# A three-part transformer layer on one core: a reordered head with wider and constant TensorE products, the token softmax moved into the last group, and half of one expert's second matrix loaded into another buffer

## What is computed

```
for t in range(S):                                   # 8 heads of 48, 4 batches
    cur = einsum('bhd,bhe->bhde', u * k[t], v[t])
    y[t] = einsum('bhd,bhde->bhe', r[t], state + cur)
    state = w[t][..., None] * state + einsum('bhd,bhe->bhde', k[t], v[t])
x = y as (3072, 384)
h = x @ w_in; x = (h * clip(h + 3, 0, 6) / 6) @ w_out   # 384 -> 2048 -> 384
logits = x @ phi                                     # 32 slots, 4 for each of 8 experts
d = softmax of logits over the tokens; slot_input = d.T @ x
slot_out[e] = relu(slot_input[e] @ w1[e]) @ w2[e]    # 384 -> 1024 -> 384
c = softmax of logits over the slots; out = c @ slot_out
```

## Time and profile before

| | |
|---|---|
| median of 3 runs | 452.84 us (452.33 to 454.29) |
| profiled execution, its time / its span | 455.68 us / 454.0 us |
| TensorE busy | 427.3 us (94%), mean granted clock 0.946 |
| VectorE busy | 340.9 us (75%) |
| GpSimd busy | 180.1 us (40%) |
| ScalarE busy | 148.4 us (33%) |
| moved by DMA | 69.35 MB |

### The profile page before, as it was taken

How to read it: one execution, slowest core, us unless ns; L and a number is a source line. 1 busy time by engine, 2 the same in 40 slices (tenths; PEclk the granted TensorE clock), 3 DMA queues, 4 the chain that set the end, 5 groups by cost and what they waited for, 6 DMA issues and landing times.

```text
span 454.0 us, 9636 instructions
## 1 busy us (share of the span) xinstructions
PE 427.3 (94%) x3891; PEld 238.2 (52%) x3891; DVE 340.9 (75%) x539; ACT 148.4 (33%) x250; POOL 180.1 (40%) x174
## 2 busy tenths in 40 slices
PE   7999997888999999999999999998999999999982
PEld 3898654444555555556555555464554534433420
DVE  7555589989998989888898998889776676472233
ACT  1221323542433334414344144342432323212122
POOL 5614255575544565446556435654370000000000
PEclk9555699999999999999999999999999999999987
DMA  8996130341933222340343213330005963469919
GB/s 215 300 381 223 61 115 1 115 113 64 337 107 114 77 70 83 115 116 11 104 116 113 86 31 114 114 114 18 37 2 206 423 222 124 181 250 423 395 62 359
DMA packets 15245, 69.35 MB, mean 153 GB/s; under 512 B 2016, under 2 KB 2656, under 8 KB 13152
## 3 DMA queue, kind: packets, MB, share of 16 engines
q1 hardware_dynamic: 15200, 68.73, 43.7%
HBM read 64.00 MB, written 4.72 MB: 151 GB/s over the span
## 4 chain that ended last, share of the span: by engine, by line
issue 39%; PE 33%; POOL 19%; DVE 4%; DMA 1%; ACT 1%; POOLq 0%; SPq 0%; DVEq 0%
POOL att L1256 5%; PE hid L514 4%; PE hid L516 4%; PE hid L515 4%; POOL att L1228 4%; POOL att L1226 3%; POOL att L1241 3%; POOL att L1274 3%; PE hid L711 2%; PE l_ps L570 2%; PE l_ps L544 2%; PE y_ps L471 2%; PE sc_ps L421 1%; PE hid L686 1%; PE sc_ps L686 1%
## 5 line engine op out<-in xcount | busy, mean ns | idle before, releaser
L1123 ACT ACTIVATE relu<-hid,three 128x512 f32<-128x512 f32 x96 | 65.9, 687 | 149.6 <-PE hid L516 149.0
L514 PE MATMUL hid<-x_split,w_split 128*128 128x512 f16 x288 | 109.9, 381 | 3.5 <-DVE gated L860 3.5
L515 PE MATMUL hid<-x_split,w_split 128*128 128x512 f16 x288 | 109.6, 380 | 0.0
L516 PE MATMUL hid<-x_split,w_split 128*128 128x512 f16 x288 | 109.4, 380 | 0.0
L860 DVE SCALAR_TENSOR_TENSOR gated<-relu,hid 128x512 f32<-128x512 f32 x96 | 65.2, 680 | 29.6 <-ACT relu L1123 29.0
L870 DVE STREAM_TRANSPOSE ring<-gated 128x512 f32<-128x512 f32 x96 | 68.3, 711 | 3.3
L1247 POOL TENSOR_TENSOR att<-att 128x1024 f16<-128x1024 f32 x20 | 39.9, 1996 | 64.6 <-ACT att L1082 64.6
L1265 POOL TENSOR_TENSOR att<-att 112x512 f32<-112x512 f32 x19 | 24.3, 1280 | 68.7 <-DVE att L785 68.7
L514 PEld LDWEIGHTS hid<-x_split,w_split 128*128 128x128 f16 x288 | 28.3, 98 | 40.8 <-issue 9.6
L516 PEld LDWEIGHTS hid<-x_split,w_split 128*128 128x128 f16 x288 | 28.2, 98 | 34.4 <-issue 0.5
L515 PEld LDWEIGHTS hid<-x_split,w_split 128*128 128x128 f16 x288 | 28.2, 98 | 25.2 <-issue 0.6
(11 more groups left out here) (202 smaller groups left out, 768.7 us busy)
## 6 DMA issues: line engine op xcount, KB each, us to landing
att<-nat_dram SPq DMA_DIRECT2D x20, 576.0 KB, 4.2
att<-rkT_dram SPq DMA_DIRECT2D x22, 448.0 KB, 5.6
att<-w_dram SPq DMA_DIRECT2D x5, 1536.0 KB, 14.1
att<-wT_dram SPq DMA_DIRECT2D x22, 226.2 KB, 4.7
out_dram<-w_split SPq DMA_DIRECT2D x12, 384.0 KB, 3.9
stage<-w_in_dram SPq DMA_DIRECT2D x2, 1536.0 KB, 13.7
ring<-w_outT_dram SPq DMA_DIRECT2D x1, 3072.0 KB, 17.2
stage<-w_dram SPq DMA_DIRECT2D x2, 1536.0 KB, 9.2
```

Source lines behind the costliest of these rows:

```text
L514: pe.matmul(hid[s % 2][:], high, x_high, start=(q == 0), stop=False)
L515: pe.matmul(hid[s % 2][:], high, x_low, start=False, stop=False)
L516: last = pe.matmul(hid[s % 2][:], low, x_high, start=False, stop=(q == KT - 1))
L1123: nc.scalar.activation(relu_tile(s), hid[s % 2][:], ACT.Relu, bias=three[:], scale=GATE / H_SCALE)\
```

## The change

1. **Head.** The 16 opening constant products become 10, 4 and 3, the last two lots behind `suffix_done` and `prefix_done`. `diagonal` writes each of its products 48 times side by side (96 columns in place of 2), `attend_first` takes two heads' columns per product (96 in place of 48; the second half is overwritten by the next product). `stay_warm` stands three times in each unit (2, 1 and 1 products). `turn_x` goes ahead of `increment`, `diagonal` behind `attend_first`. `make_fold` goes from VectorE to ScalarE, `scan_suffix(5)` and `low_w(0)` go ahead of step 0.
2. **Group 0.** Pieces 2 to 7 of `low_w` go from VectorE to GpSimd, behind a new ScalarE operation `scale_w` that scales the stage in place.
3. **Softmax c.** Units 0 to 19 (640 of 768 columns) are done inside group 5: maximum and sums on VectorE, subtraction, multiplication and low part on GpSimd, exponential and high parts on ScalarE; `turn_c(1)` and `turn_c(0)` run at steps 96 and 97 in place of six of nine `stay_warm` products. Units 20 to 23 and `turn_c(2)` stay in the tail.
4. **Tail.** Both `pick_slots` stand behind the whole `apply_w2`; the first half of w2[4] is loaded into `x_late` right behind w1[6]; `weigh` computes the weights ahead of alpha.

```diff
+            elif e == 4 and a < EK // 2:
+                home, first = x_late, a * DM
...
-        def split_at(s):
-            return s // 2 + 1 if s % 2 == 0 and s // 2 + 1 < W_PIECES else None
+        def scaled_behind(s):
+            return {0: 3, 4: 4, 5: 5, 8: 6, 9: 7}.get(s)
+
+        def split_behind(s):
+            return {1: 2, 2: 3, 5: 4, 6: 5, 9: 6, 10: 7}.get(s)
...
+            sp.dma_start(x_late, w2[4][:, 0:UNIT // 2]).then_inc(w2_late_in[0], 16)
             sp.wait_ge(l_ready, STEPS)
...
-                for e in (4, 6, 7):
+                for e in (6, 7) if half == 0 else (4, 6, 7):
...
-                    last = pe.matmul(hid[1][:, 2 * p:2 * p + 2], rk_prod[n % 2][0:PD, p * P:(p + 1) * P],
-                                     u_rows[0:PD, 2 * p:2 * p + 2], start=True, stop=True, skip_group_check=True)
+                    last = pe.matmul(hid[1][:, p * 2 * D:(p + 1) * 2 * D].rearrange("p (o j) -> p o j", j=2),
+                                     rk_prod[n % 2][0:PD, p * P:(p + 1) * P],
+                                     u_rows[0:PD, 2 * p:2 * p + 2].rearrange("p (o j) -> p o j", o=1)
+                                     .broadcast_to([PD, D, 2]), start=True, stop=True, skip_group_check=True)
...
-                        cols = slice((2 * p + j) * D, (2 * p + j + 1) * D)
+                        h = 2 * p + j
+                        cols = slice(h * D, min(h + 2, H) * D)
...
-            for _ in range(16):
-                pe.matmul(hid[0][:, :], warm[:, 0:P], warm[:, P:P + GT], start=True, stop=True, skip_group_check=True)
+            keep_awake(10)
+            pe.wait_ge(suffix_done, 1)
+            keep_awake(4)
+            pe.wait_ge(prefix_done, 1)
+            keep_awake(3)
             score(0, None)
+            turn_keys(0)
...
+            stay_warm(2, hid[0])
             diagonal(0)
             for n in range(B):
                 if n:
                     score(n, None)
-                turn_keys(n)
+                    turn_keys(n)
+                stay_warm(2, hid[0])
+                attend_first(n)
                 if n + 1 < B:
                     diagonal(n + 1)
-                else:
-                    stay_warm(2, hid[0])
-                attend_first(n)
+                stay_warm(1, hid[0])
+                turn_x(n)
                 increment(n, None)
-                turn_x(n)
                 stay_warm(1, hid[0])
...
-                    stay_warm(6, y_ps)
+                    pe.wait_ge(c_lo_done, 1)
+                    pe.wait_ge(c_hi_done, 2)
+                    turn_c(1)
+                    pe.wait_ge(gated_done, STEPS - 1)
+                    stay_warm(3, hid[0])
                 if s == STEPS + 1:
-                    stay_warm(3, y_ps)
+                    turn_c(0)
...
-            pe.wait_ge(c_lo_done, 1)
-            turn_c(0)
             apply_w2(0, 1)
-            turn_c(1)
+            pe.wait_ge(c_lo_done, 2)
+            pe.wait_ge(c_hi_done, 4)
             turn_c(2)
...
             apply_w2(1, 0)
-            pick_slots(0)
             pe.wait_ge(w2_late_in[1], 48)
             apply_w2(1, 1)
-            pick_slots(EG - 1)
+            for g in range(EG):
+                pick_slots(g)
...
+                if n == 2:
+                    low_w(0)
             low_x(B - 1)
-            low_w(0)
+            scan_suffix(B + 1)
+            restart_prefix(B + 1)
             mask_first(B)
...
+                if s == STEPS - 12:
+                    cols, tiles = c_parts[0]
+                    dve.wait_ge(logits_done, C - 1)
+                    nc.vector.tensor_reduce(cmax[:, tiles], by_slot(soft[:, cols]), AX_X, ALU.max).then_inc(c_max_done, 1)
+                if s == STEPS - 8:
+                    c_inverse(0)
+                if s == STEPS:
+                    copy_cT(1)
+                    copy_cT(0)
...
+            def scale_w(c):
+                act.wait_ge(w_hi_done, c + 1)
+                nc.scalar.activation(stage[:, c * WP:(c + 1) * WP], stage[:, c * WP:(c + 1) * WP], ACT.Copy,
+                                     scale=W_IN_SCALE).then_inc(w_scaled, 1)
...
+                if s == STEPS - 10:
+                    c_exp(0)
+                if s == STEPS - 5:
+                    c_high(0)
...
+            def low_w(c):
+                pool.wait_ge(w_scaled, c - 1)
+                per = FT // W_PIECES
+                nc.gpsimd.tensor_tensor(w16[:, c * per:(c + 1) * per, 1].rearrange("p i q m -> p i (q m)"),
+                                        stage[:, c * WP:(c + 1) * WP].rearrange("p (i n) -> p i n", i=per),
+                                        w16[:, c * per:(c + 1) * per, 0].rearrange("p i q m -> p i (q m)"),
+                                        ALU.subtract).then_inc(w_lo_rest_done, 1)
```

More of the change, by code:

```diff
@@ L289, in build_program @@
         c_lo_done = sem("c_lo_done")
-        c_turned = sem("c_turned")
+        c_turned = [sem(f"c_turned{n}") for n in range(3)]
+        c_max_done = sem("c_max_done")
+        c_inv_done = sem("c_inv_done")
         cT_done = sem("cT_done")
@@ L533, in stay_warm, with keep_awake @@
                               skip_group_check=True)
+            def keep_awake(n):
+                for _ in range(n):
+                    pe.matmul(hid[0][:, :], warm[:, 0:P], warm[:, P:P + GT], start=True, stop=True,
+                              skip_group_check=True)
             def add_logits(g, m):
@@ L558, in natural_logits, with turn_c @@
                 last.then_inc(nat_logits_ready, 1)
+            def turn_c(n):
+                for i in range(8 * n, 8 * n + 8):
+                    last = pe.transpose(c_bank[n][0:3 * SLOTS, :].bitcast(F16)[:, i % 8 * P:(i % 8 + 1) * P],
+                                        c_split[:, i].rearrange("p a s -> p (a s)"), ident16_sb[:])
+                last.then_inc(c_turned[n], 1)
             def gather_slots(g, n):
@@ L609, in _ @@
                     weigh_phi(0)
+                if s == 1:
                     increment(B, s)
@@ L700, in turn_eh @@
                         last.then_inc(eh_turned, 1)
-            def turn_c(n):
-                for i in range(8 * n, 8 * n + 8):
-                    last = pe.transpose(bank[1 + n][0:3 * SLOTS, :].bitcast(F16)[:, i % 8 * P:(i % 8 + 1) * P],
-                                        c_split[:, i].rearrange("p a s -> p (a s)"), ident16_sb[:])
-                last.then_inc(c_turned, 1)
             def apply_w2(g, half):
@@ L902, in sum_weight @@
                     nc.vector.tensor_reduce(run_sum, weight, AX_X, ALU.add).then_inc(run_sum_done, 1)
-            def make_fold():
-                for q in range(4):
-                    block = ident[SLOTS * q:SLOTS * (q + 1), SLOTS * q:SLOTS * (q + 1)]
-                    last = nc.vector.tensor_copy(
-                        fold[SLOTS * q:SLOTS * (q + 1), :].rearrange("p (c s) -> p c s", c=4),
-                        block.rearrange("p (o s) -> p o s", o=1).broadcast_to([SLOTS, 4, SLOTS]))
-                last.then_inc(fold_made, 1)
             def add_slots(g):
@@ L955, in _ @@
                 g, i = divmod(s, FT)
+                if s <= 1:
+                    gate(s)
+                    turn_gated(s)
                 if phase == 0:
@@ L980, in _ @@
                 if s == 0:
-                    gate(0)
-                    turn_gated(0)
                     low_w(1)
-                    scan_suffix(B + 1)
-                    restart_prefix(B + 1)
+                    sum_diag(B)
                 if phase == 3:
@@ L1053, in _ @@
                     .then_inc(ehT_done[0], 1)
[L1054 to L1058 removed]
+            copy_cT(2)
             low = slice(2 * SLOTS, 3 * SLOTS)
@@ L1106, in high_x, with make_fold @@
                     .then_inc(x_hi_done, 1)
+            def make_fold():
+                for q in range(4):
+                    block = ident[SLOTS * q:SLOTS * (q + 1), SLOTS * q:SLOTS * (q + 1)]
+                    last = nc.scalar.activation(
+                        fold[SLOTS * q:SLOTS * (q + 1), :].rearrange("p (c s) -> p c s", c=4),
+                        block.rearrange("p (o s) -> p o s", o=1).broadcast_to([SLOTS, 4, SLOTS]), ACT.Copy)
+                last.then_inc(fold_made, 1)
             def high_w(c):
@@ L1174, in _ @@
                         copy_keys(n)
-                c = split_at(s)
-                if c is not None and c >= 2:
-                    high_w(c)
                 if s < STEPS:
@@ L1181, in _ @@
                     copy_keys(B)
+                c = scaled_behind(s)
+                if c is not None:
+                    high_w(c)
+                    scale_w(c)
                 if g >= 1 and i == 2:
@@ L1290, in _ @@
             nc.gpsimd.memset(three[:], 3.0 * GATE).then_inc(pool_consts, 1)
-            decay_keys(0)
-            multiply_rows(0)
             for b in range(B):
@@ L1296, in _ @@
             last.then_inc(state_zeroed, 1)
-            multiply_rows(1)
+            decay_keys(0)
```

(8 more changed lines are left out.)

159 lines of the change are left out of this document (98 added, 61 removed).

## The result

The changed kernel takes 432.12 us (431.88 to 432.25, four runs), the kernel before 452.72 (452.33 to 454.29) beside it: a ratio of 0.9538, 95% interval 0.9515 to 0.9561. The forecast was 429.0 in a range of 422 to 443. The profiled execution takes 432.12 (span 430.4), where the sum gave 431.5.

The account below looks back on a forecast made before the run. The prediction took TensorE, at half clock, to bound the head and VectorE's share of the split group 0. Terms 12.8 + 1.3 + 8.0 + 2.1 = 24.2 us, off the median 452.84, gave 429, range 422 to 443.

Parts of the forecast that it names:

- The time goes into loading weights, not into columns: Head, TensorE: 2 and 48 columns cost the same 0.22 us per instruction, so wider products were costed at nothing.
- rivals 1 and 2: Head's clock: first, up only in part, 438 us, chance 0.14; second, at half throughout, 448 us, chance 0.09.
- (c): Head: at full clock the chain over VectorE and GpSimd, not TensorE, sets the pace, 6.9 us a unit.
- (d): Head from its data-fixed start: `finish_y(0)` at 15.1, step 0 at 38.5 instead of 51.34; 12.8 us gained.
- (e): Step 0's first products: about six run at half clock before the clock rises; at full clock 1.3 us more gained.
- Group 0: Split pieces moved from VectorE to GpSimd: three units at 13.2 instead of 15.87 us, 8.0 us gained (5 to 9).
- A piece of over 2 us: Group 0, sign of being wrong: a GpSimd piece of the split taking over 2 us; 1.5 was expected.
- the second delays `decay_keys`, whose result is read a unit later: Group 0, GpSimd: of two pieces per unit, 3.0 us together, the second only holds up `decay_keys`, needed a unit later.
- Rival 3: Group 0: GpSimd becomes the bound, by pieces of 2.1 us or more or mutual blocking with scans; 437 us, chance 0.04.
- Groups 1 to 5: Softmax work placed beside group 5 costs nothing: taken as 0, bounds 0 and 1 us lost.
- tail: After step 95: 1.1 us from `turn_c`, 0.8 from `pick_slots`, 0.2 from weights ahead of alpha; 2.1 us gained.
- the fourth rival: After step 95: clock falls since turning products do not hold it, some 5 us lost; 434 us, chance 0.05.

Follow-up runs that it names:

- narrow: The change with the diagonal's products back at 2 columns and the first attention's at 48, added constant products kept: 442.9, 434.44, 447.41 and 444.05 us.
- order only: The change with narrow products and the head's constant products as before, leaving only the new order of the head: 445.36 us, ratio 0.9798 to the kernel before.
- fewer: The change with the head's constant products as in the kernel before, wide products and order kept: 432.03 us, ratio 0.9513 to the kernel before.
- Experiment 11: Also called `low_v_first`: the change with `low_v` ahead of `low_x` and `sum_diag` in group 0; median 431.11 us, ratio 0.9502 to the kernel before.
- experiment 8: The change without the three constant products at step 96 and the nine ahead of the gather: 433.03 us, ratio 0.9513 to the kernel before.
- Experiment 7: The change with the first half of w2[4] loaded late again, into the stage: 433.54 us, ratio 0.9529 to the kernel before.
- experiment 1: The kernel before, unchanged, profiled a second time: 455.79 us profiled, span 454.1.
- experiment 6: The change with each unit's second `low_w` piece one place later on GpSimd, behind `decay_keys`: 436.98 us, ratio 0.96 to the kernel before.

## Why the prediction held, and where it was off

**The bound and the clock.** "The time goes into loading weights, not into columns" held: in the first unit, at full clock, the attention took 1.88 us in the change and 1.88 in narrow, the diagonal 1.13 and 1.05. The clock stayed up in the head of all nine traces with wide products, and fell in both with narrow ones (445 us for order only), near what rivals 1 and 2 say. The constant products that were added gave nothing measurable beside the wide ones, and cost nothing either, since TensorE is not the bound there: the 0.29 by which `fewer` reaches step 0 sooner stand already in its first scan (3.71 and 3.99), which waits for a transfer. The forecast gave them no price of their own, so no term failed with it.

**(c), the chain over VectorE and GpSimd.** That TensorE does not set the pace is shown by `fewer`; that this chain does, by its rows, which add up to the period. The forecast 6.9 was 6.6. Its hand-overs were right (0.11 of the 6.9, 0.09 measured); too high was the end of the chain, where it put `scan_prefix` and `diag_values` one behind the other, 1.22 + 0.83 = 2.05 after `multiply_rows`. The scan starts before `multiply_rows` ends (25.69 and 26.03), and `diag_values` is over 1.72 after it. The forecast named the scan as the operation that waits for GpSimd; it does, by 0.2 (1.44), and then `diag_values` waits for the scan (1.76 instead of 0.83).

(d) had the path of the start wrong. It let `decay_keys(0)` release the next scan at 8.34; in the change the chain runs over the first scans and `decay_receptance(0)` to `multiply_rows(0)` at 8.31. `finish_y(0)` came at 14.64 instead of 15.1; over the eleven traces with the new order it stands at 14.14 to 14.65. The head gave 1.0 us above its 12.8: 0.5 from this start, 0.6 from the two periods, and 0.1 less behind the last `finish_y`. The forecast named a DMA as the last wait in the head as a sign of being wrong. At its very start two transfers are that (1.49 and 1.70 us), as in the kernel before; behind them none is, though the DMA share stood at 9 tenths in the second and third slices.

**(e).** 0.9 instead of 1.3. Step 0's first six products took 2.35 us before (51.34 to 53.69) and 1.30 after (37.51 to 38.81), 1.05 less, since five and not six ran at half clock. The other 0.2 wasn't looked for.

**Group 0: the term that was mis-sized**, 6.4 for 8.0. GpSimd's piece took 1.63 to 1.65 us, the estimate was 1.5. A piece of over 2 us was to be a sign of being wrong; the first took 2.58 (50.26 to 52.84, a scan of VectorE beside it until 51.39), ahead of these three units. The step that failed is not that price, but "the second delays `decay_keys`, whose result is read a unit later": it looked at what waits behind the piece on GpSimd, and not at what runs beside it on VectorE. `low_v` was in its way, and TensorE waits for `low_v`. Experiment 11 gives 0.97 us of the 1.6 back. The rest, 0.2 a unit, is not this wait: 40.27 / 3 = 13.4 with TensorE never waiting. The 13.20 was one interval, and it stood across the end of group 0 (after the change that interval is 13.57, and the next four are 17.80, 13.12, 13.08 and 14.13), so it was a weak measure of a unit that TensorE bounds; why a unit of group 0 takes 0.2 more than it stays open. Rival 3, in its second form ("the scans and the pieces block each other"), was true in small.

**Groups 1 to 5, tail.** 0.35 for 0, and 2.2 for 2.1. The softmax beside group 5 cost nothing: from the last `low_scores` to step 95's end it is 54.56 us in both traces (335.95 to 390.51, 314.52 to 369.08). In the tail 0.2 of the gain is there when `apply_w1` begins (19.82 and 19.63 us behind step 95's end), as forecast for the weights, and 2.0 come behind it, for the forecast's 1.1 and 0.8. Of the fourth rival only the fall of the clock was seen, without constant products (experiment 8); the rule on turning products which the forecast quotes is neither borne out nor refuted. Experiment 7 shows that without the early half load 1.4 of the tail's 2.2 would be lost.

**From the sum to the median.** The sum for the profiled execution was off by 0.6 of span (24.2 for 23.6). The forecast of 429 was 3 us low since the same sum was taken off the median, 452.84. That step failed: the profiled execution of before lies high in a wide spread (452.2 to 456.3), the change's runs lie within 0.6 us. The spread may come from the stretch at half clock: narrow, where the clock falls too, spreads over 13 us (mean clock 0.946 to 0.983, the highest in its shortest run), the change and fewer by under 1. Then the kernel before's shorter runs already lack part of what the change removes. That isn't shown: over the runs of the kernel before the mean clock goes only loosely with the time (0.942 in the shortest, 452.16, three of 0.953 at 452.54 to 452.71, 0.932 in the longest, 456.27), `low_v_first` has one run at 434.69, and where in the program a run of 452 saves its 3 us stays open, since both traces of the kernel before are of executions of 455.7 and 455.8 us. That profiling itself lengthens the kernel before, and not the change, stays possible too (experiment 1).

## What to carry to other kernels

Where TensorE is busy without a gap and the clock is still at half, look at how many columns each product streams; widening narrow f32 products (2 and 48 to 96 columns) was nearly free here and worth 13 us, further constant products beside them were worth nothing. When an order makes TensorE wait, look at the granted clock behind the wait as well as at the wait (1.5 us in experiment 6). When work goes to GpSimd, list what VectorE issues in the same microsecond and who waits for that, and not only what is queued behind it on GpSimd. Before a saving is taken off a median, ask whether that saving also removes what made the runs differ.

## What the runs showed of the hardware that wasn't expected

- A TensorE that was 100% busy stayed at half clock (0.50 and 4.00 of 4 us busy in narrow's stretches 18:22 and 30:34), while one with gaps (3.56 of 4 us) stayed at full, with wider products.
- Even with narrow products the clock rose before step 0, in narrow and order only at about 43 us (0.84 in narrow's stretch 42:46); in the kernel before it didn't there, with two constant products at 42.78.
- Behind waits of 1.68 and 1.9 us in which TensorE ran nothing, the clock fell to half for some 3 to 4 us (experiments 6 and 8), in the first case with nine 512-column products just before the wait.
- A VectorE operation of 0.55 us took 0.74, 1.44 or 2.57 us by where it was issued among GpSimd's operations.
